# Query products and state updates crossed between batch halves for odd heads, one bank for both merge stages

## The reference, cut to what matters

```python
# B=4 batches, H=8 heads, S=768 tokens, D=48
k_n = k / (np.linalg.norm(k, axis=-1, keepdims=True) + 1e-06)
state = np.zeros((B, H, D, D))
for t in range(S):
    y[:, :, t] = q_t @ state
    v_old = k_n_t @ state
    state = state + beta_t * outer(k_n_t, v_t - v_old)
x = y.transpose(0, 2, 1, 3).reshape(B * S, H * D)        # 3072 x 384
# x goes through a mixture of 8 experts (384 -> 1024 -> 384, relu, weights P by
# 8 rounds of normalisation), and then through (h * cos(h)) @ w_out, h = x @ w_in
```

## Time and profile before

| | us |
|---|---|
| median of 3 runs | 2218.53 |
| lowest and highest | 2217.21, 2219.99 |
| the profiled execution | 2215.68 |
| its span, first to last instruction | 2213.9 |
| attention stage, to the expert passes | about 316 |

### The profile page before, as it was taken

How to read it: one execution, slowest core, us unless ns; L and a number is a source line. 1 busy time by engine, 2 the same in 40 slices (tenths; PEclk the granted TensorE clock), 3 DMA queues, 4 the chain that set the end, 5 groups by cost and what they waited for, 6 DMA issues and landing times.

```text
span 2213.9 us, 41130 instructions
## 1 busy us (share of the span) xinstructions
PE 2169.7 (98%) x15885; PEld 1793.8 (81%) x15885; DVE 1019.6 (46%) x1724; ACT 702.7 (32%) x1197; POOL 507.2 (23%) x409
## 2 busy tenths in 40 slices
PE   8798999999999999999999999999999999999999
PEld 7777778888888888888888888888888888888887
DVE  8898726432322323223223232232322347777777
ACT  4655543111111111111111111111111237666665
POOL 1000010045332322323323233232332330000000
PEclk6899999999999999999999999999999999999999
DMA  5434332021111111111111101111111100000001
GB/s 140 121 91 119 104 117 74 24 54 43 29 33 29 29 40 36 32 30 28 33 28 28 47 28 33 28 30 32 28 35 42 29 24 15 15 15 15 0 15 71
DMA packets 83116, 97.74 MB, mean 44 GB/s; under 512 B 6848, under 2 KB 68608, under 8 KB 83008
## 3 DMA queue, kind: packets, MB, share of 16 engines
q1 hardware_dynamic: 83008, 96.18, 16.0%
HBM read 82.69 MB, written 8.75 MB: 41 GB/s over the span
## 4 chain that ended last, share of the span: by engine, by line
PE 91%; DVE 6%; issue 1%; ACT 1%; DMA 0%; SPq 0%; DVEq 0%; ACTq 0%
PE h L774 7%; PE h L776 7%; PE h L775 7%; PE p_h L774 7%; PE p_h L776 7%; PE p_h L775 7%; PE am_y L812 4%; PE am_y L813 4%; PE am_y L814 4%; PE cy_y_y L812 4%; PE cy_y_y L813 4%; PE cy_y_y L814 4%; PE o_y L812 2%; PE o_y L813 2%; PE state_y L814 2%; PE state_y L812 2%
## 5 line engine op out<-in xcount | busy, mean ns | idle before, releaser
L1384 POOL TENSOR_TENSOR acc<-acc,py 128x512 f32 (+1 forms) x252 | 324.1, 1318 | 746.2 <-DVE py L1732 746.2
L1244 ACT ACTIVATE hhi<-h 128x512 fp32r<-128x512 f32 x182 | 109.0, 599 | 769.7 <-PE h L776 769.7
L1695 DVE SCALAR_TENSOR_TENSOR hlo<-h,hhi 128x512 fp32r<-128x512 f32 x182 | 125.9, 692 | 473.5 <-ACT hhi L1244 473.5
L1695 DVE SCALAR_TENSOR_TENSOR hlo<-p_h,hhi 128x512 fp32r<-128x512 f32 x182 | 125.8, 691 | 404.3 <-ACT hhi L1244 404.3
L1346 POOL TENSOR_TENSOR wlo<-stage,whi (+1 forms) x114 | 146.8, 1289 | 630.1 <-ACT whi L1089 605.2
L774 PE MATMUL p_h<-xhi,whi 128*128 (+1 forms) x690 | 269.1, 390 | 0.6 <-DVE scr L1792 0.6
L774 PE MATMUL h<-xhi,whi 128*128 (+1 forms) x690 | 268.9, 390 | 0.0
L776 PE MATMUL h<-xhi,wlo 128*128 (+1 forms) x690 | 268.7, 389 | 0.0
L776 PE MATMUL p_h<-xhi,wlo 128*128 (+1 forms) x690 | 268.7, 389 | 0.0
L775 PE MATMUL p_h<-xlo,whi 128*128 (+1 forms) x690 | 268.6, 389 | 0.0
L775 PE MATMUL h<-xlo,whi 128*128 (+1 forms) x690 | 268.6, 389 | 0.0
(11 more groups left out here) (279 smaller groups left out, 3820.6 us busy)
## 6 DMA issues: line engine op xcount, KB each, us to landing
stage<-wcat SPq DMA_DIRECT2D x38, 768.0 KB, 4.4
pb<-p_scratch SPq DMA_DIRECT2D x84, 256.0 KB, 4.7
kq<-kqt SPq DMA_DIRECT2D x48, 192.0 KB, 3.5
v<-vrow SPq DMA_DIRECT2D x24, 192.0 KB, 3.7
kb<-krow SPq DMA_DIRECT2D x24, 192.0 KB, 3.8
acc<-yT SPq DMA_DIRECT2D x144, 32.0 KB, 2.3
kT<-kta SPq DMA_DIRECT2D x20, 192.0 KB, 4.3
acc<-y_scratch SPq DMA_DIRECT2D x5, 768.0 KB, 4.7
```

The costliest lines, as they stand in the source:

```text
L1244: act.activation(hhi[:, j, :], hps[j % 2][:, 0:TILE], ACT.Relu).then_inc(s["hhi_done"], 1)
L1384: pool.tensor_tensor(y, y, py[:, d, :], ALU.add).then_inc(s["added"], 1)
L1695: dve.scalar_tensor_tensor(out=hlo[:, j, :], in0=hps[j % 2][:, 0:TILE], scalar=0.0, in1=hhi[:, j, :].bitcast(F32), op0=ALU.max, op1=ALU.su ...
```

## The change

Odd heads get their queried keys (P), their W and their rows of keys for the state on the other batch's partitions. The query products of odd heads write half b ^ 1, into a second bank (`p_ps` becomes two banks, even and odd heads), so they go round all four quarters. W's products put odd heads on the other half as well (bank and half both by `n % 2`). State products are then split: even heads, some other block, a wait for the even ones (`ku_even`), odd heads. Output products are split in the same way (`y_even`), since the two sorts write the same bank's halves from different halves. Where a step is marked `between` (not a first one, c other than 1, the next not a first one) the query products stand between even and odd output products; in first steps between even and odd state products; else where they were. The second bank for P is taken from the merges: both stages and both halves of a group's units share `am_ps`. That changes the waits of merges and of the fill products, and which banks key products, joins and early expert products use. The fill products in (0,1) move ahead of `turned(3)`. The memset of `state_ps` at the start goes. The host packs key rows of odd heads for the other half.

```diff
@@ -203,11 +203,14 @@
     cy_ps = ctx.enter_context(nc.psum_tensor("cy_y02_y10", [P, 2, 512], F32))
     y_all = cy_ps[:, :, 0:HH * CT].rearrange("p a (n i) -> p a n i", i=CT)
     chain_all = cy_ps[:, :, HH * CT:HH * (CT + HD)].rearrange("p a (n d) -> p a n d", d=HD)
-    state_ps, p_ps = ps("state_y01"), ps("p_h1")
-    am_ps = [ps("am0_y11"), ps("am1_y12")]
+
+    p_ps = ctx.enter_context(nc.psum_tensor("p_h1_y12", [P, 2, 512], F32))
+    p_all = p_ps[:, :, 0:HH * CT].rearrange("p e (a i) -> p e a i", i=CT)
+
+    state_ps, am_ps = ps("state_y01"), ps("am_y11")
     h_ps, o_ps = ps("h0"), ps("o_y00")
-    hps = [h_ps, p_ps]
-    yps = [[o_ps, state_ps, cy_ps[:, 0, :]], [cy_ps[:, 1, :], am_ps[0], am_ps[1]]]
+    hps = [h_ps, p_ps[:, 0, :]]
+    yps = [[o_ps, state_ps, cy_ps[:, 0, :]], [cy_ps[:, 1, :], am_ps, p_ps[:, 1, :]]]
 
     def sem(name):
         return ctx.enter_context(nc.semaphore(name))
@@ -215,7 +218,7 @@
...
-          "a_done a_evac p_done p_evac ext_done leaf_chain zt_done z_done sc_done m_first m_firsted sc_first m_done m_evac ks_done r_done w_done w_evac ku_done "
+          "a_done a_evac p_done p_evac ext_done leaf_chain zt_done z_done sc_done m_first m_firsted sc_first m_done m_evac ks_done r_done w_done w_evac ku_even ku_done y_even "
@@ -257,7 +260,7 @@
 
     def key_bank(g, r):
 
-        return (h_ps, o_ps, *am_ps)[r] if g < AHEAD else (h_ps, o_ps)[r % 2]
+        return (h_ps, o_ps, am_ps, state_ps)[r] if g < AHEAD else (h_ps, o_ps)[r % 2]
 
     def keyed(g, c):
 
@@ -479,7 +482,7 @@
                 pe.wait_ge(a["p_evac"], i)
             for h in range(HEADS):
                 for b in range(2):
-                    mm = pe.matmul(rows(p_ps, b)[:, h * CT:(h + 1) * CT], kq[b * CT:b * CT + HD, i % KQ, h, 0, :],
+                    mm = pe.matmul(rows(p_all, b ^ h % 2)[:, h % 2, h // 2, :], kq[b * CT:b * CT + HD, i % KQ, h, 0, :],
                                    kq[b * CT:b * CT + HD, i % KQ, h, 1, :], start=True, stop=True)
             mm.then_inc(a["p_done"], 1)
 
@@ -505,16 +508,14 @@
 
             if stg == 1:
                 pe.wait_ge(a["m_evac"], 4 * g + m)
-            elif g == 1:
-                pe.wait_ge(a["m_evac"], 4)
             else:
-                pe.wait_ge(a["m_evac"], 4 * (g - 1) + 2 * k + 2)
-            merge_units(g, stg, am_ps[k], k * 16, (k + 1) * 16).then_inc(a["m_done"], 1)
+                pe.wait_ge(a["m_evac"], 4 * g + k)
+            merge_units(g, stg, am_ps, k * 16, (k + 1) * 16).then_inc(a["m_done"], 1)
 
 
         def joins(c):
 
-            bank = h_ps if c else am_ps[0]
+            bank = h_ps if c else am_ps
             if c > 1:
                 pe.wait_ge(a["join_evac"], c)
             for n in range(HEADS):
@@ -590,9 +591,11 @@
             if t < EARLY - 1:
 
                 pe.wait_ge(o["evac"], OUTS * t + 2 + d)
-            elif d < 2:
+            elif d == 0:
 
                 pe.wait_ge(a["m_evac"], 4 * NG)
+            elif d == 1:
+                pe.wait_ge(a["p_evac"], NS)
             else:
                 pe.wait_ge(a["y_evac"], NS)
             bank = early_bank(t, d)
@@ -611,13 +614,13 @@
 
             if (g, c) in KEYS_BESIDE:
                 key_products(*KEYS_BESIDE[g, c])
+            if (g, c) in UNREAD:
+
+                pe.wait_ge(a["m_evac"], {(0, 1): 2, (0, 2): 4, (0, 3): 5, (1, 0): 7}.get((g, c), 8))
+                unread(UNREAD[g, c], am_ps)
             if (g, c) == (0, 1):
                 turned(3)
                 first_merge(2)
-            if (g, c) in UNREAD:
-
-                pe.wait_ge(a["m_evac"], {(0, 1): 2, (0, 2): 4, (0, 3): 4, (1, 0): 6}.get((g, c), 8))
-                unread(UNREAD[g, c], am_ps[1 if (g, c) == (0, 3) else 0])
             if g >= 2 and c == 0:
                 early_up(g - 2, 3)
             if g >= 2 and c == 1:
@@ -642,12 +645,31 @@
             if g >= 2 and c == 1:
                 early_down(g - 2, 1)
 
+        def state_products(c, heads, start):
+
+            for h in heads:
+                for b in range(2):
+                    mm = pe.matmul(rows(state_ps, b, HD)[:, h * HD:(h + 1) * HD], rows(kb, b ^ h % 2)[:, c, h, :],
+                                   rows(W, b ^ h % 2)[:, h ^ HH * (h % 2), :], start=(start and h == 0), stop=False, skip_group_check=True)
+            return mm
+
+        def output_products(i, odd):
+
+            for n in range(odd, HH, 2):
+                for par in range(2):
+                    for b in range(2):
+                        mm = pe.matmul(rows(y_all, b ^ par, HD)[:, par, n, :], rows(W, b ^ odd)[:, (par ^ odd) * HH + n, :],
+                                       rows(P_, b ^ odd)[:, i % 2, par * HH + n, :], start=False, stop=True, skip_group_check=True)
+            return mm
+
         def step(g, c):
             first, last = is_first(g, c), is_last(g, c)
             i = g * STEPS + c
             k_of, q_of = (lambda b, h: kq[b * CT:b * CT + HD, i % KQ, h, 0, :]), (lambda b, h: kq[b * CT:b * CT + HD, i % KQ, h, 1, :])
 
             fours = [(par * HH + n, par, n, b) for n in range(HH) for par in range(2) for b in range(2)]
+
+            between = not first and c != 1 and not (i + 1 < NS and is_first((i + 1) // STEPS, (i + 1) % STEPS))
             if i > 0:
 
                 pe.wait_ge(a["y_evac"], i)
@@ -678,9 +700,10 @@
 
             for h, par, n, b in fours:
                 r = rows(v, b ^ par)[:, c, h, :] if first else rows(R, b ^ par)[:, h, :]
-                mm = pe.matmul(rows(chain_all, b)[:, par, n, :], rows(X, b ^ par)[:, g % 2, c * HEADS + h, :], r, start=True, stop=True)
+                mm = pe.matmul(rows(chain_all, b ^ n % 2)[:, par ^ n % 2, n, :], rows(X, b ^ par)[:, g % 2, c * HEADS + h, :], r, start=True, stop=True)
             mm.then_inc(a["w_done"], 1)
-            query_products(i + 1)
+            if not first and not between:
+                query_products(i + 1)
             beside_update(g, c)
             if (g, c) == (0, 0):
                 first_merge(1)
@@ -693,22 +716,26 @@
             if c == 3 and g + 1 < NG:
                 merge(g + 1, 1)
             pe.wait_ge(a["w_evac"], i + 1)
-            if not first:
+            if not last:
+                pe.wait_ge(a[f"kb_loaded{c}"], 16 * (g + 1))
+                state_products(c, range(0, HEADS, 2), first).then_inc(a["ku_even"], 1)
+            if first:
+                query_products(i + 1)
+            else:
                 for h, par, n, b in fours:
                     pe.matmul(rows(y_all, b ^ par, HD)[:, par, n, :], rows(S, b, HD)[:, h, :], q_of(b, h), start=False, stop=False,
                               skip_group_check=True)
             if not last:
-                pe.wait_ge(a[f"kb_loaded{c}"], 16 * (g + 1))
-                for h in range(HEADS):
-                    for b in range(2):
-                        mm = pe.matmul(rows(state_ps, b, HD)[:, h * HD:(h + 1) * HD], rows(kb, b)[:, c, h, :],
-                                       rows(W, b)[:, h, :], start=(first and h == 0), stop=False, skip_group_check=True)
-                mm.then_inc(a["ku_done"], 1)
+
+                pe.wait_ge(a["ku_even"], updated(g, c))
+                state_products(c, range(1, HEADS, 2), False).then_inc(a["ku_done"], 1)
             pe.wait_ge(a["p_evac"], i + 1)
-            for h, par, n, b in fours:
-                mm = pe.matmul(rows(y_all, b ^ par, HD)[:, par, n, :], rows(W, b)[:, h, :], rows(P_, b)[:, i % 2, h, :], start=False,
-                               stop=True, skip_group_check=True)
-            mm.then_inc(a["y_done"], 1)
+            output_products(i, 0).then_inc(a["y_even"], 1)
+            if between:
+                query_products(i + 1)
+
+            pe.wait_ge(a["y_even"], i + 1)
+            output_products(i, 1).then_inc(a["y_done"], 1)
             beside_outputs(g, c)
             if (g, c) == (0, 0):
                 second_merge(1)
@@ -724,7 +751,7 @@
 
         pe.wait_ge(a["warm"], 1)
         for _ in range(5):
-            pe.matmul(p_ps[:, 0:2 * P], stage[:, 0:P], stage[:, P:3 * P], start=True, stop=True)
+            pe.matmul(p_ps[:, 0, 0:2 * P], stage[:, 0:P], stage[:, P:3 * P], start=True, stop=True)
         for m in range(2):
             key_products(0, m)
         for m in range(2):
@@ -732,21 +759,21 @@
         query_products(0)
 
         pe.wait_ge(a["zeros_made"], 1)
-        pe.wait_ge(a["zeroed"], 2)
-        unread(8, state_ps)
+        pe.wait_ge(a["zeroed"], 1)
+        unread(8, cy_ps[:, 0, :])
         for m in range(2):
             key_products(2, m)
-        unread(6, state_ps)
+        unread(6, cy_ps[:, 0, :])
 
         pe.wait_ge(a["a_evac"], 4 * AHEAD)
         pe.wait_ge(a["zt_half"], 1)
         joins(0)
-        unread(2, state_ps)
+        unread(2, cy_ps[:, 0, :])
         pe.wait_ge(a["zx_first"], 1)
         turned(0)
         joins(1)
         first_merge(0)
-        unread(1, state_ps)
+        unread(1, cy_ps[:, 0, :])
         second_merge(0)
```

(5 more changed lines are left out.)

## The result

The changed kernel takes **2225.57 us** (median of 6 runs, 2224.99 to 2228.44), the kernel before 2217.55 (6 runs, 2214.33 to 2219.99). The ratio is 1.0039, with an interval of 1.0026 to 1.0052: the change makes the kernel slower by some 8 us, where I had forecast 5.2 us less. The profiled execution took 2228.44, span 2226.7 us. Further down, single executions of 2284 to 4564 us, one each in three sets of runs, are left out of the ratios.

The account below looks back on a forecast made before the run. TensorE and VectorE alternately bound the attention stage, TensorE the later layers. Savings of 0.3 + 1.0 + 0.7 + 1.1 + 0.2 + 1.9 = 5.2 us gave a forecast of 2213.3 us, range 2208 to 2221.5.

Parts of the forecast that it names:

- (3) of "What it adds": Gap during W's copy: query products leave it; cover remains for c=0, 2, 3, saving 0.55 us; c=1 only 0.25.
- My terms for (0,3) and (1,0): TensorE's stops of 2.53 and 2.07 us, expected at the same time but before the merge: savings of 0.7 and 1.1 us.
- I am wrong if the stops move by themselves: Sign against the forecast: TensorE's stops, such as 2.53 us in (0,3) and 2.07 in (1,0), change place.
- My four end steps: (4,2), (4,3), (5,0), (5,2): cheaper query products save 0.55 us each at full clock, 2.2 us together.
- my terms up to there: Savings at the start, in (0,0) and (0,1), in (0,3) and in (1,0): 0.3, 1.0, 0.7 and 1.1 us.
- The 0.3 us at the start: Start of the kernel: dropping the memset of state_ps lets VectorE's first diagonal copy start earlier, saving 0.3 us.
- (4): (0,3) and (1,0): fill products wait for merge evictions in the shared bank; covered at 0, up to 2 us each otherwise.
- My slower rival: Merge waits in (0,3) and (1,0) exceed their cover, with longer half-clock spells: 2222 us, chance 0.12.
- (1): Output products: TensorE waits for its own even ones before the odd ones, 0.25 us where query products don't stand between.
- The middle: (1,1) to (4,1): VectorE-bound, only 0.2 us saved; distances of R of (2,1) to (4,1) unchanged.
- The end: From (4,3) on, each of four steps shorter by about 0.5 us; the end terms from (4,2) together save 1.9.
- a rival in the good direction: From 26 to 124 us a denser TensorE spends less time at the lower clock: 2210.4 us, chance 0.14.

Follow-up runs that it names:

- padded changed kernel: The changed kernel with 120 waits on a long-passed semaphore added to TensorE's list, in two places ahead of 27 us; 2225.59 us, ratio 1.0034.

## Why the prediction was wrong, step by step

**The step that failed** is (3) of "What it adds": query products leave the gap behind W, where for c=2 and c=3 "an expert block of 9 products stands there", "so the cover remains and the whole 0.55 is saved". I checked that W would be there in time, and took the new place as free. The move alone, uncrossed, costs 7.2 to 7.8 us, and the part with c=2 and c=3 costs 9.3 by its ratio (7.5 by medians), where I had put a saving.

How it costs is only in part shown. In the changed kernel's execution the loss behind R of (3,3) has the size of its half-clock blocks (6.3 us against 1.5) and its stops (5.1 against 2.6). From (1,3) to (3,3), where the clock is full up to the last block, it loses 2.8 us, with more stops and 0.5 and 0.4 us where W's copy is late. The gap of (1,2) I had to drop. And the kernel with the move alone loses as much in the median, but in its execution ahead of (1,3) and with no half-clock block behind. So that the place of the query products in c=2 and c=3 costs the 8 us is shown by the medians of four kernels (behind W everywhere, moved alone, c=0 alone, c=2 and c=3 alone); through which of stops, clock and idle time it does so, and why there are more stops, stays open. One execution of each kernel was profiled.

**The stops.** My terms for (0,3) and (1,0), 0.7 and 1.1, took the stops of 2.53 and 2.07 us there to stay at their time. In the changed kernel neither is there: TensorE goes from W's products to the merge without a stop in both steps (80.54, 81.58 and 93.51, 94.55). "I am wrong if the stops move by themselves", I had written, and they did: out of groups 0 and 1 and into the stage behind.

**The sum's sign.** My four end steps at 0.55 each rest on TensorE being the bound from (4,2) on. The block did get shorter as said. This is (4,2) of the kernel with query products behind W, against the earlier trace rows:

```profile
255.47 0.66 PE L485 MATMUL p_h_y<-kq 48*64 48x64 f32 x32
256.06 0.50 PE L563 MATMUL h<-xhi,whi 128*128 128x512 f32 x1
```

0.59 us from start to next block instead of 1.04, where I said 0.49 (15 ns a record; it is 18). So the saving is 0.45 instead of 0.55, and the mechanism is right. An estimate of 0.8 us for the block, worked out from the 60 cycles a matmul of the Trainium skill (TensorEngine Tiling (Array Packing), Performance Considerations, Instruction Overhead), lies above this row. In that execution the end is shorter, 59.78 us from R of (4,1) to R of (5,3) against 62.56, of which 1.5 is the half-clock block that only the kernel before has there; but from (1,1) to (1,3) it is 3.2 us longer. In the median the gain is not there: with everything of the change but the move, the ratio is 0.9998. Fourteen of sixteen query products left out gave 1.8 us. Ahead of (1,1) the error is in taking idle time before R in one execution as money: R of (0,2) waited 0.27 instead of 1.65, and R of (1,1) not at all, where I had said it would still wait a little. It came 1.44 us earlier; my terms up to there gave 3.1. From (1,0) to (1,1) VectorE came late by itself, 11.06 us in the changed kernel and in the one with query products behind W, a floor that I hadn't looked for: the idle times of two steps in a row don't add up. And ScalarE's copies in (1,2) kept their time (117.79 after, 117.34 before). What is gained ahead of them turned into waiting for them: the 1.44 us are gone at R of (1,3). The 0.3 us at the start isn't to be seen either: R of (0,1) is at 48.79 with query products behind W, at 48.85 before.

**Merge waits** (4): covered at 0, right. S times q of (0,3) starts at 83.95 (before 84.10; I had said by 83), and the banks alone are at 0.9999. My slower rival was to be decided at this row, and 83.95 speaks against it; the slower result has another mechanism, which none of my cases had.

**The wait on even products** (1): the idle time ahead of the odd output products, that of their weight loads, in the changed kernel (total us, times):

```profile
  PE cy_y_y L661: 2.3, 10
```

That is 0.23 each against 0.25 said. With query products behind W there are more such waits, and they cost nothing in the end, by the same 0.9998.

**The middle**: distances unchanged, said for (2,1) to (4,1). (2,0), (2,1) and (4,2) hold to 0.1 us, but (4,0) is 1.6 and (4,1) is 2.4 us longer, and (2,2) to (3,3) are 0.3 to 0.9 longer. "VectorE-bound" was true only as long as TensorE had neither more stops nor a lower clock.

**The end**: steps from (4,3) shorter by 0.5 each. (4,3) is 0.65 and (5,3) 0.5 shorter, but (5,1) is 0.8, (5,2) 0.1 and (5,0) 3.3 longer (15.52 after 12.23): its expert block at 284.94 runs at half clock behind a stop of 1.16.

```profile
284.56 0.45 PE L679 MATMUL cy_y_y<-S,kq 48*64 48x48 f32 x2 [1.16 <-issue]
284.94 0.79 PE L563 MATMUL h<-xhi,whi 128*128 128x512 f32 x1
```

**The clock.** I had it as a rival in the good direction: a denser TensorE gets its clock back sooner. I had also written that I would be wrong if lower-clock spells changed place, and that is what happened. My error was to think of groups 0 and 1 only. There the mean clock fell to 0.62 and R of (1,1) came no later; what was slower is the blocks behind 124 us. What brings the clock down for them is open: see the last section.

## What to carry to other kernels

Before taking a move of work as free, run it alone, in the old kernel and with nothing else changed. Here the cover in the old place was checked and the new place was not, and the move cost 7.2 to 7.8 us where the rest of the change cost nothing. When wide and short products alternate in a stage that TensorE sets, their order is part of the tuning: the ten blocks of query products moved in c=2 and c=3 last 0.59 us each at full clock and cost 7.5 to 9.3 together.

A pattern in one trace, idle time with a slow block behind it, is a suspect. Look for it in the kernels that lose nothing before calling it the cause: (1,2) looks the same in both. And leave most of the work out once before making it cheaper; if hardly anything is won (here 1.8 us for over 20 of TensorE), a speed-up of it has little to win in its present place. It is no strict bound, since leaving it out also empties the gap.

## What the runs showed of the hardware

Products of 64 columns over four quarters, in an order that rotates through them, start every 18 ns (0.59 us for 32 records) or 15 (0.49), over two quarters every 33 (1.04). Two independent pairs of quarters, straight and crossed, do run beside each other.

The lower clock doesn't always cost. The kernel with query products behind W has a clock of 0.62 from 26 to 124 us where before has 0.70, and its R of (1,1) comes at 101.17 against 102.89: the steps in between are held by VectorE and ScalarE too. The same level makes an expert block 1.3 to 1.9 us longer where TensorE sets the pace. So a mean clock by stage says little; what counts is which block it falls on.

Stops of TensorE with nothing released come in all these kernels in the attention stage, up to 1.8 us each behind 124 us, at other places in each kernel. No run shows what they are.

Over all traces, 14 expert blocks behind 124 us run at half clock for most of their length, and each has a stop of 0.74 us or more in the stretch of small products ahead of it. The length of the stretch alone doesn't decide: 6.53 us of it with a stop of 0.66 was followed by full clock (the move alone), 4.44 us with one of 0.74 by half clock (before). Nor does a stop alone: in the padded changed kernel the block at 283.95 is at full clock behind a stretch of 6.44 us with one of 1.32. So stops go with the lower clock in these rows; whether they bring it, together with what, no run here tells apart.
